# Moving the leaky-ReLU result of layer 1 out of PSUM and splitting it one chunk later

## The reference, cut to what matters

```
x = local_attention(q, k, v) + upsampled_attention(mean4(q), mean4(k), mean4(v))   # (2304, 512)
h = x @ w_in1;  g = maximum(0.01 * h, h);  y = g @ w_out1     # layer 1, 512 -> 2048 -> 512
h = y @ w_in2;  g = h - tanh(h);           out = g @ w_out2   # layer 2, same sizes
```

## Time and profile before

| what | value |
|---|---|
| median of 3 runs | 1005.08 us (1001.62 to 1007.11) |
| time of the profiled execution | 1007.11 us |
| its span | 1005.3 us |
| TensorE busy | 969.7 us, 96% |
| VectorE, ScalarE, GpSimd busy | 620.3, 543.7, 385.8 us |

### The profile page before, as it was taken

One profiled execution on the slowest core, in us unless ns is written; L12 is line 12 of the kernel. 1 busy time (PEld: TensorE's weight loads), 2 busy tenths in 40 slices (PEclk: granted clock), 3 DMA queues, 4 the chain that ended last, 5 costly groups with the idle time before them and its releaser, 6 DMA issues.

```text
span 1005.3 us, 19106 instructions
## 1 busy us (share of the span) xinstructions
PE 969.7 (96%) x6672; PEld 912.0 (91%) x6672; DVE 620.3 (62%) x1178; ACT 543.7 (54%) x1254; POOL 385.8 (38%) x325
## 2 busy tenths in 40 slices
PE   6778999999999999999999999999999999999997
PEld 6668999999999999999999999889899889898996
DVE  7586456755674566556323657676676676766764
ACT  2443463454534634545354667776666676766664
POOL 2642351451723514517152557633323233333232
PEclk9557999999999999999999999999999999999999
DMA  5854201220121012200200402100000000000000
GB/s 137 201 152 110 50 24 26 49 50 24 24 48 48 22 25 48 48 25 2 64 2 1 137 1 84 54 32 1 1 32 0 17 15 0 31 0 0 32 1 32
DMA packets 87221, 41.47 MB, mean 41 GB/s; under 512 B 59776, under 2 KB 80768, under 8 KB 87168
## 3 DMA queue, kind: packets, MB, share of 16 engines
q1 hardware_dynamic: 87168, 40.78, 15.3%
HBM read 36.04 MB, written 4.72 MB: 41 GB/s over the span
## 4 chain that ended last, share of the span: by engine, by line
PE 82%; ACT 4%; DVE 4%; POOL 4%; issue 2%; SPq 2%; DMA 2%; ACTq 0%; DVEq 0%; POOLq 0%
PE ph L458 13%; PE ph L460 12%; PE ph L459 12%; PE acc L487 6%; PE acc L488 6%; PE acc L489 6%; PE acc L534 6%; PE acc L535 6%; PE acc L536 6%; PE banks L368 3%; PE banks L386 2%; POOL g_lo L1016 1%; PE banks L374 1%; POOL w_lo_b L1023 1%; DMA o_stage<-in_moe_w_out_dram 1%
## 5 line engine op out<-in xcount | busy, mean ns | idle before, releaser
L1016 POOL TENSOR_TENSOR g_lo<-scratch,g_hi 128x384 fp32r<-128x384 f32 x96 | 126.0, 1312 | 258.3 <-ACT g_hi L640 258.3
L988 POOL TENSOR_TENSOR in_lo<-w_whole,in_hi 128x512 fp32r<-128x512 f32 x64 | 82.5, 1290 | 182.3 <-ACT in_hi L624 182.3
L871 DVE TENSOR_TENSOR ph<-g,ph 128x288 f32<-128x288 f32 x128 | 58.8, 459 | 148.6 <-ACT g L658 148.4
L458 PE MATMUL ph<-x_hi,w_hi_a 128*128 128x288 f32 (+1 forms) x448 | 146.1, 326 | 4.2 <-DVE x_lo L851 4.0
L460 PE MATMUL ph<-x_hi,w_lo_a 128*128 128x288 f32 (+1 forms) x448 | 141.3, 315 | 0.0
L459 PE MATMUL ph<-x_lo,w_hi_a 128*128 128x288 f32 (+1 forms) x448 | 141.2, 315 | 0.0
L658 ACT ACTIVATE g<-ph 128x288 f32<-128x288 f32 x128 | 52.5, 410 | 145.0 <-PE ph L460 145.0
L907 DVE SCALAR_TENSOR_TENSOR scratch<-scratch,ph 128x384 f32<-128x384 f32 x96 | 53.2, 554 | 110.6 <-ACT scratch L703 106.0
L993 POOL TENSOR_TENSOR out_lo<-w_whole,out_hi 128x512 fp32r<-128x512 f32 x64 | 87.2, 1362 | 47.6 <-ACT out_hi L628 47.6
L702 ACT ACTIVATE scratch<-ph 128x384 f32<-128x384 f32 x96 | 46.8, 488 | 108.3 <-PE ph L460 106.7
L458 PEld LDWEIGHTS ph<-x_hi,w_hi_a 128*128 128x128 f32 x448 | 85.5, 191 | 8.9 <-issue 4.3
(11 more groups left out here) (168 smaller groups left out, 2765.9 us busy)
## 6 DMA issues: line engine op xcount, KB each, us to landing
out_dram<-o_stage SPq DMA_DIRECT2D x18, 256.0 KB, 2.1
w_whole<-in_moe_w_in_dram SPq DMA_DIRECT2D x16, 256.0 KB, 4.4
w_whole<-in_moe_w_out_dram SPq DMA_DIRECT2D x16, 256.0 KB, 4.5
qn<-in_q_dram SPq DMA_DIRECT2D x28, 144.0 KB
kn<-in_k_dram SPq DMA_DIRECT2D x28, 144.0 KB
v4n<-in_v_dram SPq DMA_DIRECT2D x28, 144.0 KB
vw<-in_v_dram SPq DMA_DIRECT2D x28, 122.5 KB
scratch<-in_moe_w_in_dram SPq DMA_DIRECT2D x8, 256.0 KB, 2.8
```

The source lines that it names most:

```text
L458: pe.matmul(bank, whi, x_hi[:, c, 0:width], start=(c == 0), stop=False)
L988: pool.tensor_tensor(in_lo[:, f % 2, :], w_whole[:, f - KEPT, 0:DM], in_hi[:, f % 2, :].bitcast(F32), ALU.subtract).then_inc(in_lo_done, 1)
L1016: pool.tensor_tensor(g2_lo[:, f % 3, :], g2[:, f % 2, :], g2_hi[:, f % 3, :].bitcast(F32), ALU.subtract).then_inc(g_lo_done, 1)
```

## The change

The maximum is written to `g1` in SBUF in place of the PSUM bank, so `g_done` frees the bank and `hidden1` waits for that; `g1` is now freed by `g_lo_done`, and the next ScalarE write to it waits for that. Both halves of the split read `g1` instead of PSUM. On ScalarE and on VectorE the split of a chunk moves from its own iteration, behind attention slot 2f, to the next iteration, right behind that iteration's L658 or L871 and ahead of the attention slot. The number and shapes of instructions stay the same.

```diff
-                wait_from(pe, g_lo_done, n - 1)
+                wait_from(pe, g_done, n - 1)
                 hidden(ph1[:, f % 2, 0:T1], hi, lo, x1_hi, x1_lo, T1, CD * tile if f == 0 else None)
...
                         act.wait_ge(h_done, n + 1)
-                        wait_from(act, g_done, n - 1)
+                        wait_from(act, g_lo_done, n - 1)
                         act.activation(g1[:, f % 2, :], ph1[:, f % 2, 0:T1], ACT.Copy, scale=0.01)\
                             .then_inc(leak_done, 1)
                     if f == 0:
                         keep_before()
+                    if f:
+                        split_g(n - 1, f - 1, g1[:, (f - 1) % 2, :], g1_hi)
                     between(2 * f)
-                    if f < CF:
-                        split_g(n, f, ph1[:, f % 2, 0:T1], g1_hi)
                     if KEPT <= f + 2 < CF:
                         split_in(tile, f + 2)
...
-                dve.tensor_tensor(g1_lo[:, f % 3, :], ph1[:, f % 2, 0:T1], g1_hi[:, f % 3, :].bitcast(F32),
+                dve.tensor_tensor(g1_lo[:, f % 3, :], g1[:, f % 2, :], g1_hi[:, f % 3, :].bitcast(F32),
                                   ALU.subtract).then_inc(g_lo_done, 1)
...
                         dve.wait_ge(leak_done, n + 1)
-                        dve.tensor_tensor(ph1[:, f % 2, 0:T1], g1[:, f % 2, :], ph1[:, f % 2, 0:T1], ALU.max)\
+                        dve.tensor_tensor(g1[:, f % 2, :], g1[:, f % 2, :], ph1[:, f % 2, 0:T1], ALU.max)\
                             .then_inc(g_done, 1)
                     if f == 0:
                         keep_before()
+                    if f:
+                        lo_of_g1(n - 1, f - 1)
                     between(2 * f)
-                    if f < CF:
-                        lo_of_g1(n, f)
```

## The result

| | median | runs |
|---|---|---|
| before | 1004.51 us | 4, 1001.62 to 1007.11 |
| after | 1017.4 us | 4, 1016.67 to 1022.43 |

The ratio is 1.0147, 95% interval 1.0124 to 1.0171. The medians of four runs each are 12.9 us apart, and by the ratio it is 14.8 us; all 16 runs of the changed kernel on record, these four among them, have a median of 1019.05 us. So the change costs about 13 to 15 us. The forecast of 1004.9 was wrong, and the time lies beyond the upper end of its range, 1014.

What follows compares the result with a forecast made beforehand. The TensorE, busy 96% of the span, was taken as the bound. Tile 7's -0.8, its end's +0.3 and the mixed tiles' +0.3 sum to -0.2 us, hence 1004.9 us against the 1005.08 median; 8-in-10 range 1001 to 1014.

Steps and rivals of the forecast that it cites:

- The bound: Whole kernel: TensorE busy 96% of the span; what the change speeds up is not waited for in tiles 0 to 6.
- The operands: Split reading SBUF: high part's 3 us of ScalarE time hidden; low part's collisions up to 1.3 us each, within slack, 0.
- The third rival: Mixed tiles: low part waits for several GpSimd instructions, some 3 us beyond slack in each of six, +18, 1023; chance 0.10.
- The second rival: Second attention pass: early `in_lo` follows `out_lo`, L829 loses its turn, 1.1 us in six tiles, +6.6, 1011.5; chance 0.20.
- the +0.05 a tile that was forecast for L829: First attention pass of mixed tiles: L829 ends about 0.4 us later, nearly all within slack; 0.05 x 6 = +0.3 us.
- Tile 7: Tile 7's chunks: ScalarE-VectorE loop of 2.5 us opens, some 1.7 us lost to turns: -0.8 us, bounds -2.5 and +2.0.
- Its end: End of tile 7: split of chunk 15 slips behind `out_hi` and meets the last `out_lo`, +0.3 us.
- The bank wait: `hidden1` waits for the maximum, not the low part; earlier, but it wasn't waited for, so 0.
- the later split: `down1` needs a low part made one chunk later; 1.8 us of slack left in an unmixed tile, so 0.
- the collision of `x_lo` with `out_lo` stayed: Ends of mixed tiles: this collision stays, since `x_hi` waits for work the change doesn't touch.

Runs made afterwards that it cites:

- The probe: A separate kernel, not the reference's computation: one VectorE instruction against five GpSimd ones, varying the first one's partitions and the operands; VectorE's took 0.45 to 6.32 us.
- the gap: Changed kernel plus one wait of GpSimd for its own L977 before its next instruction; 1005.88 us against 1003.78 before the change, ratio 1.0022.
- the 128 partitions: Changed kernel with GpSimd's L977 on 128 partitions instead of 96, no wait added; 1006.76 us against 1003.42 before the change, ratio 1.0033.
- the kernel with gap and hold: Changed kernel plus the wait behind L977, and `in_hi` held until the same chunk's maximum; 1003.37 us against 1003.42 before the change, ratio 0.9997.
- the two kernels that keep the old place: Operands in SBUF and bank freed by the maximum, split in its own iteration as before: without the wait behind L977 ratio 1.0047, with it 1.0016.
- the old place and the gap: Operands in SBUF, bank freed by the maximum, split in its own iteration, wait behind L977; 1004.96 us against 1003.42 before the change, ratio 1.0016.

## Why the prediction was wrong

**The bound** was read rightly: the TensorE bounds the kernel, and what the change sped up was not waited for in mixed tiles.

**The operands: the step that failed.** The prediction said: "The new low part is contiguous, so I take the first: each collision costs it up to 1.3 us, inside the 1.8 us of slack, so 0." It compared a win in layer 2 with a loss in tile 3 and put the difference down to the broadcast operand. The probe shows that this operand isn't what starves VectorE (1.15 us without it and 1.44 with it behind 128 partitions, 5.96 and 6.32 behind 96). What differed was GpSimd: in layer 2 its instructions at that place all had 128 partitions, while the row that L808 met at 326.55 had L970 with 72 at its head, which ended at 326.17. In the kernel before:

```profile
324.61 1.56 POOL L970 TENSOR_TENSOR vd<-vd,v4n 72x256 f32<-72x256 f32 x2
```

In the changed kernel the low part met L977 with 96, in every mixed tile. Of the 2.78 us a mixed tile loses, 1.93 are this (69.92 to 67.99, the same by the gap and by the 128 partitions); with tile 5's 3.45 that is 11.2 us from tile 1 on, and by the ratios, tile 0 included, 12.5 us. So the term that the prediction put at 0, the low part's collisions, is where most of the loss lies. The third rival, "the low part is starved too", had the wait and its place, with 3 us a tile where 1.93 were measured and a chance of only 0.10, but not the cause: it took the run without gaps for enough, which the 128 partitions show it is not.

**The second rival** was half right. `in_lo` did come early and L829 started behind `out_lo`. But L829 got its turn: 1.95 us, not 2.9, and L374 had no wait. The next low part waited instead, and that cost 0.46 us a tile rather than 1.1. That too was inside the step above: the prediction held each collision against the 1.8 us of slack by itself, and here two came in a row.

**The remaining 0.39 us** (2.78 - 1.93 - 0.46) is placed in part. In the kernel with gap and hold the TensorE has no wait in a mixed tile beyond the 0.33 us for `x_lo` that it had before. Counted from the tile's L851 (284.54 before, 279.80 with the hold), `hidden1` starts 0.04 us late behind the first attention pass, 0.22 late at 37.8 us, and 0.38 late at 57. The first is the +0.05 a tile that was forecast for L829. The second step arises here, first the kernel before, then the one with the hold (its L781 is L780):

```profile
320.18 0.46 DVE L780 COPY kT<-banks 128x288 f32<-128x288 f32 x1
321.06 1.23 PE L368 MATMUL banks<-kT,q_diag 128*128 128x70 f32 x10
```

```profile
315.85 0.46 DVE L781 COPY kT<-banks 128x288 f32<-128x288 f32 x1
316.44 1.33 PE L368 MATMUL banks<-kT,q_diag 128*128 128x70 f32 x10
```

The low part now stands ahead of the copy that L368 needs, which ends 0.4 us later in the tile and only 0.13 us before L368 starts; L368 starts 0.12 late and takes 0.10 longer. So 0.18 us a tile belong to the low part's new place in VectorE's order, as read from the traces; the two kernels that keep the old place don't show it. The last 0.15 us, between 49 and 57 us into the tile, isn't explained. With the old place and the gap, the 0.48 us of turns alone all fall in that same stretch.

**Tile 7** was better than forecast between chunks 6 and 15: 31.20 to 29.51, which is -1.7 where I took -0.8. ScalarE's row of chunk 15 in the changed kernel:

```profile
597.63 0.41 ACT L658 ACTIVATE g<-ph 128x288 f32<-128x288 f32 x1 [0.96 <-PE ph L460]
```

Its end was worse: from L658 of chunk 15 to L851 it is 3.83 us (597.63 to 601.46), before 2.67 (588.36 to 591.03), +1.2 where I had +0.3. The two misses cancel in good part, and that the tile's gain of 0.3 lies near the forecast 0.5 is luck. Tile 6, which I had at 0, gained 0.4, and the start of layer 2, which the sum left out, gained 0.5.

**The bank wait** at 0 and **the later split** at 0 were summed as if independent. The sum holds only for both: the later split without the release costs 25 us. With the release the slack was real, 1.70 us in a chunk of tile 6 (the low part ends at 515.09, `down1` starts at 516.79); the TensorE never waited for a low part in tile 6, and the collision of `x_lo` with `out_lo` stayed, as forecast.

## What to carry to other kernels

Where VectorE is given a second SBUF operand, look at what GpSimd runs at that time, and above all whether a GpSimd instruction on fewer than 128 partitions stands in a row without gaps, with the next one ready before it ends: then VectorE's wait isn't one instruction but can be the rest of the row. Hold the sum of collisions in a row against the slack, not each by itself. An operand in PSUM, a wait of GpSimd for itself, or 128 partitions avoids it. When one row of a trace shows a win and another a loss, list everything that differs between them, on both engines, before one difference is made the rule; and where a change pays in one stage and costs in another, make it in the first alone.

## What the hardware showed that I had not expected

- Two SBUF operands on VectorE against 128-partition GpSimd instructions: one whole instruction each in turn (1.15 us for a 0.45 us subtraction). The Trainium skill (SBUF — State Buffer, Who interferes with whom) calls the shared port pair an exclusive lock held for the whole instruction, and says that an instruction of VectorE with at most one SBUF input, outside the modes of VectorE that use both port pairs, doesn't contend. Both agree with the runs (1.15 us, and 0.45 with an operand in PSUM). One SBUF operand isn't always enough, though: L838, a scalar add on 96x3, took 1.14 us beside `in_lo` where it takes 0.17 undisturbed; which mode it ran in, no run here shows.
- A GpSimd instruction on 96 or 72 partitions, with full ones ready right behind it: VectorE waits for all of them (5.96 us for five). Here the same page and the measurement differ: by the page VectorE would get the lock after the first instruction, and it didn't. Argued and not shown: the Trainium skill (GPSIMD Engine Reference, Instruction dispatch) says that each of GpSimd's eight cores serves its own 16 partitions and begins the next instruction as soon as its share is done. The cores that a partial instruction leaves idle would then be inside the next one when the others finish, and there would be no moment at which all are free. The low part that got its turn behind L970, whose next instruction was ready only 0.1 us before its end, would fit that as well. In the kernel a gap of 0.07 us is enough.
- A wait that is met 0.14 us before its matmul is due still isn't free: 0.37 us for that matmul in place of 0.29, and 3.27 us a chunk in place of 3.18.
